# Attention and routing stage of a fused kernel: who issues the scatters, the counts, the state updates and the first transposes, and in which order

## The chip, the cores and the metric

The kernel runs on one core of a Trainium2 chip. The metric is the device time of one execution in microseconds (us). The engines are TensorE (PE), VectorE (DVE), ScalarE (ACT), GpSimd (POOL) and SyncE (SP), which here only issues DMAs.

## The reference, cut to what matters

Attention with a decay in place of a softmax (4 batches, 8 heads, 576 positions, 64 wide), then a layer of 8 experts of which each token takes the two with the best noisy logits, then a dense layer with h * cos(h).

```
ret = scores * Dmat[None, :, :, :]          # gamma ** (i - j), i >= j
x = (ret @ v).transpose(0, 2, 1, 3).reshape(B * S, H * D)      # 2304 x 512
noisy_logits = x @ w_gate + np.log1p(np.exp(x @ w_noise)) * noise
top2 = np.argpartition(-noisy_logits, 2, axis=1)[:, :2]
...
        h = np.maximum(x[mask] @ w1[e], 0.0)
        out[mask] += top2_w[mask, k, None] * (h @ w2[e])
...
h = x @ w_in
return ((h * np.cos(h)) @ w_out)
```

## The kernel before, in words

The first stage walks over 18 tiles `t` of 128 tokens (two sequences share nine tiles; within one, a running `state` carries what earlier tiles left). It is written as a software pipeline by step `s`. In step `s` PE computes the scores of tile `s` (line 1194), then for tile `s - 1` the part from the state (1209), the part from the tile itself (1217, counted in the semaphore `out_done`) and the state's growth (1225, `u_done`), then for tile `s - 2` the gate logits (1240) and the transposed rows (1245). DVE masks the scores (`scale`, line 909, result `ret`), and turns the growth into the new state (`carry`, 917). POOL multiplies q and k by decays (`q_dec`, 549, and `k_dec`, 557). ACT copies the output of a tile out of PSUM (`xT`, 634, and `x_sb`, 641). Scores of tile `t` need `ret` of tile `t - 1` done, since they write the same banks.

Routing runs beside it, in five groups of tiles (0-3, 4-7, 8-11, 12-14, 15-17). For a group, ACT does a softplus; DVE the first choice (8 small operations, lines 842-857), the second choice (7, lines 842-864) and the running sums (`sum_picks`, 869, one per tile, ending in `picked_done`); PE a small matmul that ranks the tokens (`count`, 1174-1179, ending in `counted`); and DVE the slots (`place_rows`, 881-895, ending in `pos_done`). Every one of these small DVE operations waits for the one before it. Tables such as `COUNT_AT` say in which step each runs. Then POOL scatters the rows of `x_sb` to the slots of their experts in memory, two indirect DMAs per tile (535), tiles 0 to 7 between its multiplications (`SCATTER_AT`), tiles 8 to 17 behind them. Eight transfers of zeros to the end of the experts' slots (`zero_tail`, 382) must have landed before the first scatter. SP issues the loads of qk, kv and raw weights in one fixed order; `load_qk(11)` waits until `q_dec` of tile 10 is done. Weights are split into a high and a low part as they come (ACT 608, DVE 820).

Behind the stage stands unit 0 of the experts. It is worked in two parts, its first two blocks of 128 slots (from tiles 0 to 7) ahead of the other three, which need all scatters done. Per block PE transposes the gathered rows (1270), ACT and DVE split them (`x_high` 650, `x_low` 999), then come the first product (`first1`, 1322) and the second (`first2`, 1334) for eight chunks of weights. `keep_clock(8)` (1261) is eight matmuls whose result nobody reads. After that the other units and the dense layer follow, 862 us that the change doesn't touch.

## Time and profile before

| | us |
|---|---|
| median of 3 runs | 1009.87 (1009.67 to 1010.83) |
| the profiled execution's own time | 1012.63 |
| its span, first to last instruction | 1010.7 |
| PE busy | 982.1 (97%) |
| DVE / ACT / POOL busy | 482.3 / 426.0 / 118.2 |

The profiled execution is 2.76 us longer than the median of the timed ones, and 1.93 us of it lie outside the span. Times in the trace count from the span's start. PE's weight loads run beside its matmuls and aren't added to its busy time. "Idle before" stands in brackets at a row's end, with what ended it.

### The profile page before, as it was taken

The numbers are of one execution on the slowest core, as the hardware profiler recorded it, in microseconds if no ns is written. First come the engines' busy times: TensorE is split into PE (matmuls) and PEld (weight loads), VectorE is DVE, ScalarE is ACT, GpSimd is POOL, SyncE is SP. The second block draws the span as 40 slices with busy tenths as digits, with TensorE's granted clock in tenths as the row PEclk, the third lists the DMA queues.
The fourth block names the chain that finished last, engine by engine and source line by source line (L and its number), as shares of the span: only waits on it lengthen the run. The fifth ranks groups of instructions, "written<-read, shape, count | busy, mean of one in ns | idle before, by whom it ended". The sixth has DMA issues, their size and how long they took to land.

```text
span 1010.7 us, 17316 instructions
## 1 busy us (share of the span) xinstructions
PE 982.1 (97%) x6116; PEld 887.9 (88%) x6116; DVE 482.3 (48%) x928; ACT 426.0 (42%) x779; POOL 118.2 (12%) x122
## 2 busy tenths in 40 slices
PE   8989799999999999999999989999999999999997
PEld 7878689899898989989899989999999999999996
DVE  3685464434333333333333466555555555555554
ACT  1442434333333333333334465455555555555554
POOL 4375520000000000000000131101000001010000
PEclk9996899999999999999999999999999999999999
DMA  9985552525445172544524452101010011011000
GB/s 364 308 304 208 194 202 84 197 96 177 156 129 203 62 257 75 185 147 145 187 74 148 159 192 95 42 32 42 21 52 21 21 52 37 36 34 29 31 0 32
DMA packets 64359, 122.02 MB, mean 121 GB/s; under 512 B 5696, under 2 KB 31552, under 8 KB 64320
## 3 DMA queue, kind: packets, MB, share of 16 engines
q1 hardware_dynamic: 58080, 101.05, 29.4%
q0 software_dynamic: 6240, 20.45, 6.1%
q8 instruction: 25, 0.41, 0.2%
q14 instruction: 14, 0.11, 0.0%
HBM read 83.73 MB, written 37.75 MB: 120 GB/s over the span
## 4 chain that ended last, share of the span: by engine, by line
PE 86%; DVE 4%; DMA 4%; issue 2%; SPq 1%; ACT 1%; another core or an unknown queue 1%; ACTq 0%; DVEq 0%
PE ps L1448 20%; PE ps L1467 20%; PE ps L1284 15%; PE ps L1302 14%; PE ps L1322 3%; PE ps L1334 3%; PE ps L1397 2%; PE ps L1409 2%; PE ps L1270 2%; DMA gath<-x_slots 2%; PE ps L1209 1%; PE ps L1240 1%; PE ps L1217 1%; DMA y_slots<-y_sb 1%; PE ps L1194 1%
## 5 line engine op out<-in xcount | busy, mean ns | idle before, releaser
L1284 PE MATMUL ps<-xs,w_hi 128*128 (+1 forms) x784 | 182.9, 312 | 0.0
L1020 DVE TENSOR_TENSOR w_lo<-raw,w_hi 128x1024 fp32r<-128x1024 f32 x48 | 58.8, 1225 | 170.0 <-ACT w_hi L665 170.0
L1284 PEld LDWEIGHTS ps<-xs,w_hi 128*128 128x128 f32 x784 | 133.1, 188 | 0.8
L1448 PE MATMUL ps<-x_hi,w_hi 128*128 (+1 forms) x384 | 130.8, 341 | 0.1
L1448 PE MATMUL ps<-x_hi,w_lo 128*128 (+1 forms) x384 | 129.1, 336 | 0.0
L1448 PE MATMUL ps<-x_lo,w_hi 128*128 (+1 forms) x384 | 129.1, 336 | 0.0
L790 ACT ACTIVATE turns<-ps 128x384 f32<-128x384 f32 x96 | 47.2, 491 | 183.7 <-PE ps L1448 183.6
L1284 PE MATMUL ps<-xs,w_lo 128*128 (+1 forms) x392 | 121.2, 309 | 0.0
L1144 DVE TENSOR_SCALAR turns<-turns 128x384 f32<-128x384 f32 x96 | 37.3, 388 | 167.6 <-ACT turns L790 167.6
L1467 PE MATMUL ps<-w_hi,g_hi 128*128 128x512 f32 x288 | 112.6, 391 | 2.1 <-DVE g_lo L1155 2.1
L1467 PE MATMUL ps<-w_hi,g_lo 128*128 128x512 f32 x288 | 113.3, 393 | 0.0
L1467 PE MATMUL ps<-w_lo,g_hi 128*128 128x512 f32 x288 | 113.3, 393 | 0.0
L665 ACT ACTIVATE w_hi<-raw 128x1024 fp32r<-128x1024 f32 x48 | 50.8, 1059 | 139.1 <-PE ps L1302 108.0
L1302 PE MATMUL ps<-w_hi,hs_lo 128*128 128x512 f32 x245 | 96.2, 393 | 0.0
L1302 PE MATMUL ps<-w_lo,hs_hi 128*128 128x512 f32 x245 | 96.2, 393 | 0.0
L1302 PE MATMUL ps<-w_hi,hs_hi 128*128 128x512 f32 x245 | 95.6, 390 | 0.0
L659 ACT ACTIVATE hs_hi<-ps 128x320 fp32r<-128x320 f32 x98 | 42.7, 437 | 80.9 <-PE ps L1284 80.9
L1448 PEld LDWEIGHTS ps<-x_hi,w_hi 128*128 128x128 f32 x384 | 72.1, 188 | 3.6 <-issue 0.5
L1448 PEld LDWEIGHTS ps<-x_hi,w_lo 128*128 128x128 f32 x384 | 72.1, 188 | 3.1
L1284 PEld LDWEIGHTS ps<-xs,w_lo 128*128 128x128 f32 x392 | 73.7, 188 | 0.8
L580 POOL DMA_INDIRECT y<-y_slots,pos_now x42 | 42.0, 1000 | 275.3 <-PE ps L1384 265.9
L1448 PEld LDWEIGHTS ps<-x_lo,w_hi 128*128 128x128 f32 x384 | 72.0, 188 | 0.0
(169 smaller groups left out, 1674.9 us busy)
## 6 DMA issues: line engine op xcount, KB each, us to landing
raw<-weights SPq DMA_DIRECT2D x80, 512.0 KB
y_slots<-zeros_sb SPq DMA_DIRECT2D x42, 256.0 KB, 3.7
gath<-x_slots SPq DMA_DIRECT2D x40, 256.0 KB, 3.5
y_slots<-y_sb SPq DMA_DIRECT2D x40, 256.0 KB, 2.1
qk<-qk SPq DMA_DIRECT2D x18, 512.0 KB
kv<-kv SPq DMA_DIRECT2D x18, 512.0 KB, 6.2
out<-out_sb SPq DMA_DIRECT2D x18, 256.0 KB, 2.1
x_slots<-zeros_sb SPq DMA_DIRECT2D x8, 256.0 KB, 8.2
```

The costliest lines, as they stand in the source:

```text
L580: nc.gpsimd.indirect_dma_start(out=y[j][:, :], out_offset=None, in_=y_slots, in_offset=bass.IndirectOffsetOnAxis(ap=pos_now[:, k, j:j + 1] ...
L659: nc.scalar.activation(hs_hi[:, par, half * HALF:(half + 1) * HALF], ps[5 + half][:, 0:HALF], ACT.Relu).then_inc(relu_done, 1)
L665: nc.scalar.activation(w_hi[:, f * CHUNK:(f + 1) * CHUNK], raw[:, f % 2, :], ACT.Copy).then_inc(hi_done, 1)
L790: nc.scalar.activation(turns[f % 2][:, :], h_bank(f)[:, 0:TB], ACT.Copy, scale=PER_TURN, bias=ROUND).then_inc(turn_done, 1)
L1020: tt(w_lo[:, at], raw[:, f % 2, :], w_hi[:, at].bitcast(F32), ALU.subtract).then_inc(split_done, 1)
L1144: ts(whole[:, :], whole[:, :], -ROUND, None, ALU.add).then_inc(whole_done, 1)
L1284: last_one = nc.tensor.matmul(ps[5 + half][:, 0:HALF], w[:, at:at + P], xs[:, bass.ds(g % 2, 1), a, k, half * HALF:(half + 1) * HALF].rear ...
L1302: last_one = nc.tensor.matmul(ps[j][:, :], a[:, f % 2, j * BLK:(j + 1) * BLK], w[:, at:at + DM], start=f == 0 and i == 0, stop=f == FE - 1 ...
L1322: last_one = nc.tensor.matmul(ps[5 + i % 2][:, 0:cols.stop - cols.start], w[:, at:at + P], xs[:, 0, a, k, cols], start=k == 0 and n == 0, ...
L1334: last_one = nc.tensor.matmul(ps[j][:, :], a[:, f % 2, j * BLK:(j + 1) * BLK], w[:, at:at + DM], start=f == 0 and n == 0, stop=f == FE - 1 ...
L1448: last_one = nc.tensor.matmul(h_bank(f)[:, 0:TB], w[:, cols], a[:, bass.ds(par, 1), k, :].rearrange("p a s -> p (a s)"), start=k == 0 and ...
L1467: last_one = nc.tensor.matmul(ps[j][:, :], a[f2 % 2][:, rows], w[:, cols], start=f2 == 0 and i == 0, stop=f2 == FT - 1 and i == 2)
```

## The change

Nothing is computed differently; the order changes on four engines, and two choices of PSUM bank.

- POOL: the two scatters of a tile no longer follow each other behind both multiplications; one stands behind `q_dec` and one behind `k_dec`, and all of them run one step earlier (from step 9). The zeros go out up to two steps earlier.
- DVE: `carry` comes right behind `scale`; the second choice, the sums and the slots follow it. `place_rows` of groups 0, 1, 2 stands one step earlier (8, 12, 16), that of group 3 behind `x_low` of unit 0; the first choice of group 4 moves behind `x_low` too.
- PE: `count` of groups 0, 1, 2 moves from the end of steps 8, 12, 16 to right behind their scores. The transposes of x for unit 0's first two blocks move from behind the stage into its last step, ahead of the logits of tile 17. `keep_clock` does four matmuls in place of eight. `count` of group 4 moves one product later.
- ACT: `x_high` of these blocks moves ahead of the last softplus.

The tables and the banks:

```
-COUNT_AT = {8: 0, 12: 1, 16: 2, 18: 3}
-PLACE_AT = {9: 0, 13: 1, 17: 2, 19: 3}
-SCATTER_AT = {10: (0,), 11: (1,), 12: (2,), 13: (3,), 14: (4,), 15: (5,), 16: (6,), 17: (7,)}
-ZERO_AT = {t: t - 3 for t in range(3, 3 + E)}
-SPLIT_AT = {4: 0, 5: 1, 8: 2, 9: 3, 12: 4, 16: 5}
+COUNT_AT = {8: 0, 12: 1, 16: 2}
+PLACE_AT = {8: 0, 12: 1, 16: 2}
+SCATTER_AT = {9: 0, 10: 1, 11: 2, 12: 3, 13: 4, 14: 5, 15: 6, 16: 7}
+ZERO_AT = {3: (0,), 4: (1,), 5: (2, 3), 6: (4, 5), 7: (6,), 8: (7,)}
+SPLIT_AT = {4: 0, 5: 1, 8: 2, 9: 3, 13: 4, 16: 5}
...
-            return ps[j] if isinstance(g, int) and g == 0 else ps[7]
+            return ps[j if j < FRONT[0] else j + 3] if isinstance(g, int) and g == 0 else ps[7]
...
+        def h_first(f, part_no):
+
+            return ps[(2, 5)[part_no] + f % 2]
```

POOL's walk over the tiles:

```
+                if t == 9:
+                    pool.wait_ge(x_zero, 16 * E)
+                if t in SCATTER_AT:
+                    scatter_rows(SCATTER_AT[t], 0)
                 if c < CB - 1:
...
-                if t == 10:
-                    pool.wait_ge(x_zero, 16 * E)
-                for n in SCATTER_AT.get(t, ()):
-                    scatter_rows(n)
+                if t in SCATTER_AT:
+                    scatter_rows(SCATTER_AT[t], 1)
```

ACT's step:

```
                 if t == NT - 1:
+                    for j in range(FRONT[0]):
+                        x_high(0, j)
                     softplus(NG - 1)
```

DVE's walk, and what follows it:

```
-            for s in range(NT + 2):
+            for s in range(NT + 1):
                 if s < NT:
                     scale(s)
-                if s in SECOND_AT:
-                    second_choice(SECOND_AT[s])
-                if s in PLACE_AT:
-                    place_rows(PLACE_AT[s])
                 if 0 < s <= NT and (s - 1) % CB < CB - 1:
                     carry(s - 1)
                 if s in SECOND_AT:
+                    second_choice(SECOND_AT[s])
                     sum_picks(SECOND_AT[s])
+                if s in PLACE_AT:
+                    place_rows(PLACE_AT[s])
...
-            first_choice(NG - 1)
             for j in range(FRONT[0]):
                 x_low(0, j)
+            place_rows(NG - 2)
             h_low_first(0, 0)
+            first_choice(NG - 1)
+            h_low_first(1, 0)
             second_choice(NG - 1)
             sum_picks(NG - 1)
-            h_low_first(1, 0)
+            h_low_first(2, 0)
             place_rows(NG - 1)
```

PE's step, and what follows the stage:

```
+                if s in COUNT_AT:
+                    count(COUNT_AT[s])
                 t, c = s - 1, (s - 1) % CB
...
                 t = s - 2
+                if t == NT - 1:
+                    for j in range(FRONT[0]):
+                        transpose_x(0, j)
...
-                if s in COUNT_AT:
-                    count(COUNT_AT[s])
+                if t == NT - 2:
+                    count(NG - 2)
...
-                if i == 1:
-                    pe.wait_ge(ranked, NG - 1)
...
-            for j in range(FRONT[0]):
-                transpose_x(0, j)
-            keep_clock(8)
+            keep_clock(4)
             first1(0, 0)
             first1(1, 0)
             first2(0, 0)
             first1(2, 0)
-            count(NG - 1)
             first2(1, 0)
+            count(NG - 1)
```

The order on PE around step 12, first before (from the last matmuls of step 11; the lines are those named above):

```order
L1217 MATMUL ps<-ret,kv 64x128 x8
L1225 MATMUL ps<-kv,k_dec 64x64 x8
L1240 MATMUL ps<-wg,xT 128x16 x4
L1245 MATMUL ps<-table_sb,xT 128x128 x4
L1174 MATMUL ps<-picked,table_sb 128x32
L1176 MATMUL ps<-before_sum,table_sb 128x32
L1179 MATMUL ps<-before_sum,table_sb 128x8
L1194 MATMUL ps<-qk 128x128 x8
L1209 MATMUL ps<-q_dec,state 64x128 x8
L1217 MATMUL ps<-ret,kv 64x128 x8
```

And after the change, whose lines are numbered some twenty higher (1212 the scores, 1183 to 1188 the count, 1229 and 1237 the tile's output, 1245 the state's growth, 1263 and 1268 logits and rows):

```order
L1212 MATMUL ps<-qk 128x128 x8
L1183 MATMUL ps<-picked,table_sb 128x32
L1185 MATMUL ps<-before_sum,table_sb 128x32
L1188 MATMUL ps<-before_sum,table_sb 128x8
L1229 MATMUL ps<-q_dec,state 64x128 x8
L1237 MATMUL ps<-ret,kv 64x128 x8
L1245 MATMUL ps<-kv,k_dec 64x64 x8
L1263 MATMUL ps<-wg,xT 128x16 x4
L1268 MATMUL ps<-table_sb,xT 128x128 x4
L1212 MATMUL ps<-qk 128x128 x8
```

The three matmuls of the count have gone from behind the rows of step 12 to between its scores and the output of tile 11.

POOL's list in the middle of the scatters, first before, one tile's four instructions and what follows:

```order
L535 DMA x_slots<-x_sb,pos_x 20480x512 [waits x_done,pos_done]
L535 DMA x_slots<-x_sb,pos_x 20480x512
L549 TENSOR_TENSOR q_dec<-qk,attn_table 128x512 [waits out_done,qk_in0]
L557 TENSOR_TENSOR k_dec<-kv,attn_table 128x512 [waits u_done,kv_in0]
L535 DMA x_slots<-x_sb,pos_x 20480x512 [waits x_done,pos_done]
L535 DMA x_slots<-x_sb,pos_x 20480x512
L549 TENSOR_TENSOR q_dec<-qk,attn_table 128x512 [waits out_done,qk_in1]
```

And after (552 is `q_dec`, 564 `k_dec`, 538 the scatter):

```order
L552 TENSOR_TENSOR q_dec<-qk,attn_table 128x512 [waits out_done,qk_in2]
L538 DMA x_slots<-x_sb,pos_x 20480x512 [waits x_done,pos_done]
L564 TENSOR_TENSOR k_dec<-kv,attn_table 128x512 [waits u_done,kv_in2]
L538 DMA x_slots<-x_sb,pos_x 20480x512 [waits x_done,pos_done]
L552 TENSOR_TENSOR q_dec<-qk,attn_table 128x512 [waits out_done,qk_in0]
L538 DMA x_slots<-x_sb,pos_x 20480x512 [waits x_done,pos_done]
L564 TENSOR_TENSOR k_dec<-kv,attn_table 128x512 [waits u_done,kv_in0]
```

The two multiplications no longer stand side by side; a scatter stands ahead of each.

The end of the stage on PE, first before, from step 18 on:

```order
L1209 MATMUL ps<-q_dec,state 64x128 x8
L1217 MATMUL ps<-ret,kv 64x128 x8
L1240 MATMUL ps<-wg,xT 128x16 x4
L1245 MATMUL ps<-table_sb,xT 128x128 x4
L1174 MATMUL ps<-picked,table_sb 128x24
L1176 MATMUL ps<-before_sum,table_sb 128x24
L1240 MATMUL ps<-wg,xT 128x16 x4
L1245 MATMUL ps<-table_sb,xT 128x128 x4
L1270 MATMUL ps<-table_sb,gath 128x128 x8
L1261 MATMUL ps<-w_hi 128x512 x8
L1322 MATMUL ps<-xs,w_hi 128x256
```

And after (1197 is the transposes of x, 1284 the four matmuls of `keep_clock`, 1334 the first product):

```order
L1229 MATMUL ps<-q_dec,state 64x128 x8
L1237 MATMUL ps<-ret,kv 64x128 x8
L1263 MATMUL ps<-wg,xT 128x16 x4
L1268 MATMUL ps<-table_sb,xT 128x128 x4
L1183 MATMUL ps<-picked,table_sb 128x24
L1185 MATMUL ps<-before_sum,table_sb 128x24
L1197 MATMUL ps<-table_sb,gath 128x128 x8
L1263 MATMUL ps<-wg,xT 128x16 x4
L1268 MATMUL ps<-table_sb,xT 128x128 x4
L1284 MATMUL ps<-w_hi 128x512 x4
L1334 MATMUL ps<-xs,w_hi 128x256
```

The transposes of x now stand ahead of the logits and rows of tile 17, which come between them and the first product.

## Rows read from the trace of the kernel before

**Rows 1.** Windows view of six stretches; per engine busy us (instructions).
```profile
core 0: us, PE busy (x) PEld busy (x) DVE busy (x) ACT busy (x) POOL busy (x), PEclk, DMA share, GB/s
36.94:42.02 5.08, 5.08 (x78) 4.55 (x77) 4.67 (x15) 1.63 (x4) 1.85 (x2) 1.00 1.03 356
61.41:106.42 45.01, 38.67 (x467) 34.80 (x467) 28.88 (x68) 15.86 (x27) 29.23 (x28) 0.81 0.68 241
76.79:92.97 16.18, 14.76 (x122) 13.16 (x124) 9.46 (x30) 2.35 (x4) 7.67 (x8) 0.50 0.59 210
106.42:122.89 16.47, 10.30 (x76) 8.76 (x76) 7.01 (x34) 5.15 (x10) 10.36 (x11) 0.79 0.56 213
122.89:148.74 25.85, 24.43 (x163) 22.11 (x163) 17.02 (x66) 8.16 (x15) 9.53 (x9) 1.00 0.51 187
148.74:1010.70 861.96, 850.71 (x4592) 770.00 (x4592) 394.24 (x675) 373.45 (x691) 44.32 (x49) 1.00 0.29 96
```

**Rows 2.** Timeline of PE, 36.9 to 58 us: start, length, engine, line, operation.
```profile
36.94 1.16 PE L1194 MATMUL ps<-qk 64*128 64x128 f32 x16
...
39.97 0.64 PE L1225 MATMUL ps<-kv,k_dec 128*64 128x64 f32 x16
...
47.15 0.39 PE L1176 MATMUL ps<-before_sum,table_sb 128*128 128x32 f32 x2
...
56.33 1.16 PE L1194 MATMUL ps<-qk 64*128 64x128 f32 x16
```

**Rows 3.** Waits of PE, 0 to 125 us: total us, times, longest.
```profile
PE ps L1194 <- DVE ret L909: 4.5, 2, 3.0
...
PE ps L1209 <- DVE state L917: 3.1, 3, 1.6
```

**Rows 4.** Timeline of DVE, 59 to 93 us.
```profile
60.52 2.77 DVE L846 TENSOR_TENSOR hots<-t_b,code 128x32 f32<-128x32 f32 x1
...
63.90 0.76 DVE L869 TENSOR_TENSOR before_sum<-before_sum,picked 128x8 f32<-128x8 f32 x4
...
69.79 4.03 DVE L820 TENSOR_TENSOR w_lo<-raw,w_hi 128x1024 fp32r<-128x1024 f32 x1 [2.62 <-ACT w_hi L608]
...
91.08 0.18 DVE L862 SCALAR_TENSOR_TENSOR t_c<-hots,logit 128x32 f32<-128x32 f32 x1
...
92.42 0.19 DVE L864 TENSOR_TENSOR picked<-hots 128x32 f32<-128x32 f32 x1
```

**Rows 5.** Timeline of POOL, 50 to 64 us.
```profile
50.83 1.27 POOL L549 TENSOR_TENSOR q_dec<-qk,attn_table 128x512 f32<-128x512 f32 x1 [2.81 <-PE ps L1217]
...
59.96 0.97 POOL L535 DMA_INDIRECT x_slots<-x_sb,pos_x  x1 [0.30 <-issue]
60.95 1.29 POOL L549 TENSOR_TENSOR q_dec<-qk,attn_table 128x512 f32<-128x512 f32 x1
62.17 1.06 POOL L557 TENSOR_TENSOR k_dec<-kv,attn_table 128x512 f32<-128x512 f32 x1
63.40 1.01 POOL L535 DMA_INDIRECT x_slots<-x_sb,pos_x  x1 [0.17 <-issue]
```

**Rows 6.** Timeline of the SP queue, 50 to 146 us.
```profile
52.17 0.33 SPq L389 DMA_DIRECT2D qk<-qk  x1
...
141.31 2.23 SPq L423 DMA_DIRECT2D gath<-x_slots  x5
```

**Rows 7.** Timeline of PE, 112 to 149 us.
```profile
119.32 2.51 PE L1261 MATMUL ps<-w_hi 128*128 128x512 f32 x8
...
144.48 1.03 PE L1270 MATMUL ps<-table_sb,gath 128*128 128x128 f32 x8
145.27 0.47 PE L1334 MATMUL ps<-w_hi,hs_hi 128*128 128x512 f32 x1
```

**Rows 8.** Timeline of ACT, 106 to 123 us.
```profile
111.92 0.60 ACT L634 ACTIVATE xT<-ps 128x512 f32<-128x512 f32 x1 [5.02 <-remote]
```

**Rows 9.** Timeline of DVE, 109 to 123 us.
```profile
117.62 0.20 DVE L886 TENSOR_TENSOR pos_hot<-hots,ps 128x48 f32<-128x48 f32 x1 [7.64 <-remote]
```

More of the change, by code:

```diff
@@ L417, in _ @@
                     load_chunk(SPLIT_AT[t + 1], SPLIT_AT[t + 1])
-                if t in ZERO_AT:
-                    zero_tail(ZERO_AT[t])
+                for e in ZERO_AT.get(t, ()):
+                    zero_tail(e)
             load_chunk(FE - 2, FE - 2)
@@ L529, in _, with scatter_rows @@
             nc.gpsimd.memset(zeros_sb[:, :], 0.0).then_inc(rows_zero, 1)
-            def scatter_rows(t):
+            def scatter_rows(t, k):
                 pool.wait_ge(pos_done, group_of(t) + 1)
                 pool.wait_ge(x_done, t + 1)
-                for k in range(2):
-                    nc.gpsimd.indirect_dma_start(
-                        out=x_slots, out_offset=bass.IndirectOffsetOnAxis(ap=pos_x[:, k, t:t + 1], axis=0),
-                        in_=x_sb[t][:, :], in_offset=None).then_inc(rows_early if t < EARLY else rows_late, 16)
+                nc.gpsimd.indirect_dma_start(
+                    out=x_slots, out_offset=bass.IndirectOffsetOnAxis(ap=pos_x[:, k, t:t + 1], axis=0),
+                    in_=x_sb[t][:, :], in_offset=None).then_inc(rows_early if t < EARLY else rows_late, 16)
             for t in range(NT):
@@ L624, in softplus, with x_high @@
                     nc.scalar.activation(sin_ready[:, :], tab("half_pi"), ACT.Exp)
+            def x_high(g, j):
+                act.wait_ge(tx_done, TPU * g + j + 1)
+                nc.scalar.activation(
+                    xs[:, bass.ds(g % 2, 1), 0, :, j * BLK:(j + 1) * BLK].rearrange("p a k s -> p (a k) s"),
+                    x_bank(g, j)[:, :].rearrange("p (k s) -> p k s", k=KD_TILES), ACT.Copy).then_inc(xs_hi_done, 1)
             def step(s):
@@ L679, in relu_first @@
                     act.wait_ge(p2_done, i - 1)
-                nc.scalar.activation(hs_hi[:, f % 2, cols], ps[5 + i % 2][:, 0:cols.stop - cols.start], ACT.Relu
+                nc.scalar.activation(hs_hi[:, f % 2, cols], h_first(f, part_no)[:, 0:cols.stop - cols.start], ACT.Relu
                                      ).then_inc(relu_done, 1)
@@ L1049, in _ @@
             for f in range(2, FE):
[L1050 removed]
+                if f > 2:
+                    h_low_first(f, 0)
                 if f == 2:
@@ L1181, in count, with transpose_x @@
                 last_one.then_inc(counted, 1)
+            def transpose_x(g, j):
+                pe.wait_ge(gath_in[j], 16 * g + 16)
+                if not isinstance(g, int) or g > 0:
+                    pe.wait_ge(xs_done, TPU * g + j)
+                for k in range(KD_TILES):
+                    last_one = nc.tensor.transpose(x_bank(g, j)[:, k * BLK:(k + 1) * BLK], gath[j][:, k * P:(k + 1) * P],
+                                                   ident)
+                last_one.then_inc(tx_done, 1)
             def step(s):
@@ L1263, in _ @@
             pe.wait_ge(split_done, 1)
-            def transpose_x(g, j):
-                pe.wait_ge(gath_in[j], 16 * g + 16)
-                if not isinstance(g, int) or g > 0:
-                    pe.wait_ge(xs_done, TPU * g + j)
-                for k in range(KD_TILES):
-                    last_one = nc.tensor.transpose(x_bank(g, j)[:, k * BLK:(k + 1) * BLK], gath[j][:, k * P:(k + 1) * P],
-                                                   ident)
-                last_one.then_inc(tx_done, 1)
             def product1(g, f):
@@ L1339, in first2 @@
                         last_one.then_inc(y_ready, 1)
-            for j in range(FRONT[0]):
-                transpose_x(0, j)
-            keep_clock(8)
+            keep_clock(4)
             first1(0, 0)
@@ L1347, in _ @@
             first1(2, 0)
+            first2(1, 0)
             count(NG - 1)
-            first2(1, 0)
             for f in range(3, FE):
```

14 lines of the change are left out of this document (4 added, 10 removed).

## The prediction

> **What bounds the kernel now.** I read the windows view first: the stage that the change touches, and its hand-over to the experts. Behind 148.74 us there are 862 us with PE busy for 850.7 and a granted clock of 1.00 [rows 1]; nothing that the change moves stands there, so its time counts only if PE reaches that point earlier. In the stage PE is the bound while nothing disturbs it: one step lasts 5.08 us, with PE busy for 5.08 [rows 1]. From 61.41 to 106.42, steps 12 to 17, it took 45.01 us. Six undisturbed steps and two counts would take 6 x 5.08 + 0.5 + 0.7 = 31.7; a count costs about 0.5 or 0.7 (one starts its second matmul pair at 47.15 and takes 0.39 more, beside the first pair; the one of step 12 has three) [rows 1, 2]. So 13.3 us were lost, in two forms. The waits view has PE waiting for `ret` (4.5 us in 2 waits) and for `state` (3.1 in 3) [rows 3]. And behind the longest of these, 3.0 us up to 76.79, the granted clock is 0.50 from 76.79 to 92.97, the lower level of 1.2 GHz, while PE is busy for 14.76 of 16.18 us [rows 1]: at 2.4 GHz that work is 7.4 us, so the slow stretch alone cost 7.4.
>
> What made DVE late is seen in its timeline beside POOL's. A small operation (`hots`) that starts at 60.52 takes 2.77 us, where its like takes 0.19; a split that starts at 69.79 takes 4.03 [rows 4]. POOL runs a scatter to 60.93, `q_dec` to 62.24 and `k_dec` to 63.23 without a gap; 63.29 is where DVE's operation ends, and only then comes POOL's next scatter, after 0.17 us [rows 5]. DVE is shut out while POOL's multiplications follow each other, and already in the scatter ahead of them. The sums at 63.90 (0.76 for four) run beside a scatter unhindered [rows 4, 5]: a scatter that no multiplication follows doesn't shut it out.
>
> The rule for this is in the Trainium skill, SBUF — State Buffer, Who interferes with whom: an operation of VectorE with two SBUF inputs and one of GpSimd exclude each other, and the one that starts first has the ports for its whole instruction. By that rule alone the longest hold is one multiplication, 1.29 us, and each of the two later counts below would wait 0.5 us less (1.1 us held instead of 1.6); the gain would be 8.4 us in place of my 7.4. This trace differs, with 2.77 us and 4.03 us, so the sum goes by the trace.
>
> **The change part by part.**
>
> *GpSimd alternates.* The hold of 2.77 us falls apart into two: scatter and `k_dec`, scatter and `q_dec`. Each lasts from the middle of the scatter (0.4 us into it: the operation at 60.52 was 0.56 in) to the end of the multiplication, 0.57 + 1.06 = 1.6 and 0.57 + 1.29 = 1.9 us [rows 4, 5]. No single hold is as long as before, but together they are 3.5 us of a cycle of some 4.7 (60.95 + 1.22 + 1.23 + two scatters of 1.27), where it was 2.9. DVE's free stretches are 0.6 us each, enough for two or three small operations.
>
> *State first.* The waits for `state`, 3.1 us, go: the small operations now stand behind `carry`. `ret` stands as before, except that the slots of group 1 now end ahead of the long `ret` of tile 13. With the shorter holds I give the six steps their 31.7 us, that is 13.3 us back, and charge the waits that come anew.
>
> *Counts behind the scores.* This is the cost. The count needs the sums, and these now come after `carry`. In a step the state's growth starts 3.03 us in (39.97 - 36.94) [rows 2]; `carry` ends 4.1 us in. `q_dec` begins where the tile's output ends, some 3.4 us in, and lasts 1.27 [rows 5], so the second choice gets going 4.6 us in. It takes 1.53 (91.08 to 92.61) and the sums 0.76 [rows 4]: 6.9, or 1.9 into the next step, while PE is through with the scores at 1.1 (the length in [rows 2]). So the count of group 0, where no scatters run, makes PE wait 0.9. For groups 1 and 2 a scatter and `k_dec` come in between: DVE gets 0.6 us in, is held for 1.6 and ends 3.5 us into the step: 2.4 us of waiting, for each. Lower bound 0.9; upper bound 5, if POOL runs late and a second and third hold are met. I take 2.4 twice. Together 5.7. PE has nothing else to do meanwhile, since it works in order; behind the count are queued the output of the tile, and with it `xT` on ACT and POOL's next `q_dec`.
>
> *Scatters a step earlier.* POOL at tile 9 now waits for the slots of group 0 (about 49.3: step 8 starts at 42.02, the wait of 0.9 and the count of 0.5 put the growth of tile 7 at 47.1, then come `carry` and seven operations like those of the choices). Behind that wait stand one scatter, `k_dec`, another scatter and `q_dec` of tile 10, 1.27 + 1.05 + 1.27 + 1.3 = 4.9 us. That `q_dec` ran from 50.83 and released SP's `load_qk(11)` at 52.17; the scores of tile 11 started at 56.33, 4.2 us later [rows 2, 5, 6]. Now it goes out at 54.3, and the scores start at 58.4 instead of 56.33 + 0.9 (the wait already charged): 1.2 us more. Bounds 0 and 3.5.
>
> *Zeros earlier, split later.* At most two transfers of 256 KB more stand ahead of the loads of tiles 7 to 10. PE didn't wait for any of these, and I charge nothing; if the cover is gone it is 1 us. For `ret` and scores that a hold or the split delays I add 0.9.
>
> *The end of the stage.* From 106.42 to the first product at 122.89 it took 16.47 us, with PE busy for 10.30 at a clock of 0.79 [rows 1]. In the new order PE does there step 18 without scores (1.1) and growth (0.5), 3.5 us, with a count, 0.5; eight transposes, 0.8 (144.48 to 145.27); the logits and rows of tile 17, 1.5 (what a step has behind its growth); and four matmuls of `keep_clock`, 1.2 (eight took 2.51) [rows 2, 7]. That is 7.5 us, and the split of x on ACT and DVE hides behind the last two. So up to 9.0 us are to be had. But part of the 16.47 was no order of ours: ACT sat idle for 5.02 us before `xT` of tile 17, and DVE 7.64 before the slots of group 3, both put down to "remote", that is to nothing that the trace shows as running [rows 8, 9]; the matmuls that they waited for stand in the timeline some us before. POOL was issuing eight scatters in a row then, and will again. Bounds for this lateness 0 and 7.6; I keep the middle of the two rows, 6.3. That leaves 2.7 us.
>
> *Behind it.* The slots of group 4 come one `first2` later (1.4 us), and with them the last scatters and the five loads that SP issued at 141.31; PE took them up at 144.48 without waiting [rows 6, 7]. Between 0 and 1.4, I take 0.8.
>
> **The sum.** 13.3 - 5.7 - 1.2 - 0.9 + 2.7 - 0.8 = 7.4 us. The profiled execution took 1012.63, so 1005.2; it is 2.8 above the median of the timed runs, which gives 1002.4.
>
> **The rivals.**
>
> *The slow clock comes again.* A wait of 3.0 us led to it before, one of 1.6 at 62.5 did not. My waits at the counts are 2.4, in between, and there are two. For it: the wait for `ret` up to 76.79 wasn't alone, others preceded it; against: steps on either side are fully busy. Price 7.4, the whole gain: 1009.8.
>
> *The picks are cut to pieces (slower).* The place is the second choice of groups 1 and 2. If POOL runs a little late, the free stretches of 0.6 us let two or three of its eleven operations through at a time, and each count waits 5 us. Two times 2.6 more, and such a wait surely brings the slow clock: 7.4 - 5.2 - 7.4 = -5.2, or 1015.1. It decides as soon as the clock falls and the two counts together wait 2 us longer than the 4.8 that I say. Against it: POOL depends on PE's output, so while PE waits, POOL runs dry and frees DVE.
>
> *The lateness at the end is gone.* The transposes need only the loads, and logits stand behind them. Then 6.3 more: 996.1. Against it: the same scatters in a row.
>
> **How the numbers follow.** Forecast 0.40 (its own range 999 to 1006), slow clock 0.32, cut picks 0.14, lateness gone 0.09, and 0.05 for the rest. The range from 997 to 1012 leaves out about 0.18. A change within 0.2%, 2 us, can't be told from none by this measurement. The forecast and the third case are faster, and of the slow-clock case, which lies at the edge of that band, a third is faster, half the same and the rest slower: faster 0.62, same 0.17, slower 0.21.
>
> **What would show it.** Right: no operation of DVE above 2 us between 50 and 95; PE's waits at 1183 some 1 and twice 2.4 us; no wait at 1229 for `state`; a clock of 1.00 to 95; the first product at about 115. Wrong: a wait above 3 us at a count with a clock of 0.5 behind it; a start of the first product later than 120; or new waits behind 149, where I expect the same 862 us.

## The result, and the profile after

The kernel after took 1015.11 us (median of 6 runs, 1013.07 to 1016.94) against 1009.79 for the kernel before (6 runs): a ratio of 1.0047, 95% interval 1.0033 to 1.0062. In a second set of runs it was 1.0046 (1.0028 to 1.0065). The forecast was 1002.4, in a range up to 1012; the time lies outside it, on the slower side. The profiled execution of after took 1014.13 us, with a span of 1012.2.

The windows view of after, first the stages of [rows 1] (steps 8 to 11, steps 12 to 17, the end of the stage, the first part of unit 0, the rest), then three stretches at a low clock. The columns are the length, the busy time of PE, PE's weight loads, DVE, ACT and POOL, then the granted clock, the DMA share and GB/s:

```profile
41.76:65.79 24.03, 21.09 (x277) 18.61 (x276) 13.64 (x40) 9.85 (x16) 14.53 (x13) 0.93 0.69 251
65.79:108.05 42.26, 36.03 (x467) 32.13 (x466) 28.81 (x72) 14.98 (x26) 25.92 (x23) 0.88 0.68 239
108.05:120.56 12.51, 9.70 (x73) 8.35 (x73) 5.06 (x24) 5.43 (x12) 5.23 (x6) 0.76 0.45 176
120.56:148.90 28.34, 25.40 (x164) 22.32 (x162) 18.36 (x74) 8.41 (x16) 12.11 (x12) 0.98 0.52 183
148.90:1012.20 863.30, 851.09 (x4592) 769.85 (x4592) 394.60 (x675) 373.46 (x691) 45.57 (x49) 1.00 0.30 96
59.15:63.70 4.55, 4.55 (x48) 4.00 (x50) 1.29 (x2) 0.00 (x0) 4.13 (x4) 0.62 1.02 383
69.70:73.40 3.70, 3.70 (x36) 3.35 (x37) 0.64 (x2) 0.00 (x0) 0.00 (x0) 0.57 0.42 169
93.25:100.90 7.65, 5.97 (x53) 5.29 (x55) 3.79 (x14) 0.00 (x0) 1.74 (x2) 0.56 0.65 236
```

Steps 8 to 11 took 24.03 us, where from 42.02 to 61.41 it was 19.39 [rows 1]. Steps 12 to 17 took 42.26 instead of 45.01, the end of the stage 12.51 instead of 16.47, the first part of unit 0 28.34 instead of 25.85, the rest 863.30 instead of 861.96 [rows 1]. Ahead of step 8, which begins at 41.76 instead of 42.02, 0.26 us were won, so this is 4.64 - 2.75 - 3.96 + 2.49 + 1.34 - 0.26 = 1.5 us, the difference of the two spans. The one long stretch at half clock is gone, and three short ones have come: 0.62, 0.57 and 0.56 are mixtures of the levels 1.2 and 2.4 GHz.

PE's waits from 41 to 110 us (total, times, longest), the line before the colon, and two of them in its timeline:

```profile
PE ps L1183 <- DVE before_sum L875: 4.6, 3, 2.2
PE ps L1212 <- DVE ret L915: 2.3, 2, 2.0
PE ps L1212 <- DMA qk<-qk: 2.3, 1, 2.3
```

```profile
69.20 0.41 PE L1183 MATMUL ps<-picked,table_sb 128*128 128x32 f32 x2 [2.24 <-DVE before_sum L875]
...
93.25 1.31 PE L1212 MATMUL ps<-qk 64*128 64x128 f32 x16 [1.96 <-DVE ret L915]
```

The waits for `state` [rows 3] are gone. In their place stand three at the counts (L1183: 0.65, 2.24 and 1.67 us) and one for the load of `qk` of tile 11. DVE's longest operations between 50 and 95:

```profile
65.89 1.78 DVE L850 TENSOR_TENSOR t_b<-t_a,table_sb 128x32 f32<-128x32 f32 x1
...
82.32 2.48 DVE L826 TENSOR_TENSOR w_lo<-raw,w_hi 128x1024 fp32r<-128x1024 f32 x1 [2.21 <-ACT w_hi L614]
...
89.79 2.00 DVE L852 TENSOR_TENSOR hots<-t_b,code 128x32 f32<-128x32 f32 x1
```

The 2.77 and 4.03 us of [rows 4] are gone too, but a choice of 0.19 us still takes 1.8 or 2.0, and there are more of these.

The hand-over, in POOL's timeline (eight scatters, then six for group 3 and six for group 4; the first of each six is shown), SP's and PE's:

```profile
120.13 0.95 POOL L538 DMA_INDIRECT x_slots<-x_sb,pos_x  x1 [5.83 <-DVE pos_x L901]
...
131.34 1.77 POOL L538 DMA_INDIRECT x_slots<-x_sb,pos_x  x1 [3.93 <-DVE pos_x L901]
```

```profile
141.46 2.23 SPq L427 DMA_DIRECT2D gath<-x_slots  x5
```

```profile
144.28 1.25 PE L1197 MATMUL ps<-table_sb,gath 128*128 128x128 f32 x8 [1.53 <-DMA gath<-x_slots]
...
148.90 0.45 PE L1334 MATMUL ps<-xs,w_hi 128*128 128x384 f32 x1 [1.41 <-DVE xs L1005]
```

POOL waits 5.83 us for the slots of group 3 and 3.93 for those of group 4. The gather loads go out at 141.46, where it was 141.31 [rows 6], and PE now waits 1.53 us for them. So the 2.3 us by which the first product begins earlier are lost at the second part, which starts at 148.90 instead of 148.74. Of the 2.49 us by which the first part is longer, 1.53 are this wait, and 0.97 are a longer busy time of PE (25.40 against 24.43), at a clock of 0.98 in place of 1.00.

### The profile page after: what moved, and what is told of

Its sections match the earlier page's. It is cut to its first block, busy times and chain, and to the rows that moved or that the text cites. A ratio compares the mean times of both kernels' runs of the same rounds, so it can differ in the third digit from the quotient of the medians.

```text
span 1012.2 us, 17321 instructions
## 1 busy us (share of the span) xinstructions
PE 982.5 (97%) x6112; PEld 886.8 (88%) x6112; DVE 480.5 (47%) x928; ACT 425.7 (42%) x779; POOL 122.1 (12%) x122
## 4 chain that ended last, share of the span: by engine, by line
PE 83%; DMA 5%; issue 4%; DVE 3%; POOL 2%; SPq 1%; ACT 1%; ACTq 0%; POOLq 0%; DVEq 0%
PE ps L1458 20%; PE ps L1477 19%; PE ps L1298 15%; PE ps L1316 14%; DMA gath<-x_slots 2%; PE ps L1197 2%; PE ps L1334 2%; PE ps L1407 2%; PE ps L1346 2%; POOL x_slots L538 2%; PE ps L1419 2%; DMA y_slots<-y_sb 1%; PE ps L1237 1%; PE ps L1229 1%; PE ps L1212 1%
```

## The experiments

The runs were made in five sets, each on one chip and beside runs of the kernel before on that chip, so each ratio stands for itself. The medians of before in them were 1010.39 us (b_pool, b_tail, a_table, a_pool), 1003.46 (before2, t_chain, b_chain, a_q11), 1011.18 (after2, a_cend, a_chain, t_alt), 1010.70 (a_warm, b_cnt, t_altz, best1) and 1010.01 (a_warm2, best2). A difference of 0.001 in a ratio is 1 us. Where two ratios come from different sets, the chip differs as well as the kernel, and the text says what the traces show beside them.

**A second trace of before.** The forecast was built on one trace whose own time lay 2.8 us above the median.

> The kernel before, once more, for a second trace. If the first trace was a usual execution, the span is 1010 to 1011 and steps 12 to 17 take 45 us with 16 us at half clock; if it was a long one (its own time is 2.8 us above the median), the span is 1007 to 1009 and these steps take 41 to 43.

It took 1005.18 us, with a span of 1003.3, on a chip where the median of before was 1003.46. The span lies below both of the expected ones. Its windows: steps 12 to 17, the end of the stage, the first part of unit 0, the rest, and the only stretch at half clock:

```profile
61.80:103.03 41.23, 33.87 (x467) 30.53 (x467) 28.83 (x68) 15.87 (x27) 29.32 (x28) 0.92 0.75 267
103.03:113.39 10.36, 8.30 (x77) 7.04 (x77) 7.26 (x34) 5.15 (x10) 7.92 (x9) 1.00 0.70 256
113.39:139.11 25.72, 24.31 (x162) 21.95 (x163) 16.96 (x66) 8.16 (x15) 11.98 (x12) 1.00 0.58 210
139.11:1003.30 864.19, 851.07 (x4592) 769.88 (x4592) 394.43 (x675) 373.28 (x691) 44.59 (x49) 1.00 0.29 96
77.22:86.77 9.55, 7.19 (x77) 6.46 (x77) 5.51 (x18) 1.74 (x3) 5.44 (x6) 0.64 0.56 203
```

Steps 12 to 17 took 41.23 us, within the second of the expected ranges. This alone doesn't settle the question, since the chip is another one and this execution too was longer than the median there. But b_tail and b_chain below leave the order of these steps as in before, and b_tail ran on a chip of the usual speed, in an execution as long as its median (1010.93 and 1011.0 us). Its steps 12 to 17:

```profile
61.73:103.16 41.43, 34.09 (x467) 30.71 (x467) 29.03 (x68) 15.86 (x27) 29.15 (x28) 0.92 0.72 261
```

In b_chain they took 40.96. The undisturbed length was 31.7, so a usual execution loses 9.3 to 9.7 us there and not 13.3. In before2 the slow stretch is 9.55 us long and not 16.18, and costs 7.19 x (1 - 0.64) = 2.6 us and not 7.4. The rest varies by itself: 864.19 here, 861.96 before, 863.30 in after.

**One part alone, and one part undone.** b_pool and b_tail put a part into before; a_table and a_pool take one out of after.

```diff
 b_pool: before, tile loop of GpSimd
+                if t in SCATTER_AT:
+                    scatter_rows(SCATTER_AT[t], 0)
                 if c < CB - 1:
...
+                    scatter_rows(SCATTER_AT[t], 1)
 a_pool: after, the same lines taken out, and both scatters behind k_dec
 a_table: after with
+COUNT_AT = {8: 0, 12: 1, 16: 2, 18: 3}   (at the steps' ends)
+PLACE_AT = {9: 0, 13: 1, 17: 2}
+SCATTER_AT = {10: 0, 11: 1, ... 17: 7}   (zeros and splits in the steps of before too)
 b_tail: before with the diff's parts behind step 17 on PE, ACT and DVE
```

> Before, with one part of the change alone: at tiles 10 to 17 each scatter stands behind one multiplication, the tables of before kept. Timetable theory (the loss of 5.3 us comes from counts, slots and scatters a step earlier): this stays near before, 1007 to 1011, DVE's operations of 2.77 and 4.03 us gone, the half clock not longer than the 16 us of before. Alternation theory (the rival: scatters between the multiplications cost GpSimd or DVE more than they free): 1013 to 1016, with DVE's picks cut into more pieces and PE waiting for ret more than 4.5 us.

> Before, with the end of the stage alone changed: the x tiles of unit 0 transposed ahead of the last logits, their banks, four instead of eight clock-keeping products, rows placed and experts chosen behind the first slots of unit 0. Timetable theory: 1008 to 1011; the first product begins 1 to 5 us earlier than 122.89, and the second part of unit 0 still begins near 148.9, since the rows of group 4 reach their slots no earlier. Hand-over theory (rival: the new end is the loss): 1013 to 1016, the second part at 151 or later.

> After, with the tables of before (counts at the end of steps 8, 12, 16, places and scatters a step later); alternation, state first and the new end stay. Timetable theory: 1006 to 1010, 5 to 9 us less than after; no wait for the load of qk at step 11, no wait of PE at a count, half clock under 10 us between 41 and 107. Alternation or hand-over theory: stays at 1013 to 1016.

> After, with both scatters of a tile behind both multiplications again, one step earlier than before. Timetable theory: 1013 to 1017, the waits at the counts and for the load of qk at step 11 stay, unless the second multiplication, now ahead of the wait for the slots, lets the load go out by 53 (then 2 us less). Alternation theory: 1009 to 1011.

Measured: b_pool 1.0027 (1.0013 to 1.0042), b_tail 1.0010 (0.9998 to 1.0022), a_table 1.0042 (1.0026 to 1.0057), a_pool 1.0038 (1.0019 to 1.0058). My theory at that point, that the earlier tables are the loss, fell in its simple form: without them (a_table) the kernel stays slow, and alternation alone costs 2.8 us. The new end costs nothing that can be measured, and gains nothing. State first had no run of its own; what is left for it, 1.0042 less the 1.0027 and 1.0010 of the other two parts, is 0.0005, within the error. But a_pool shows that alternation isn't the whole loss either: after without it is at best 0.9 us faster, which is within the error. Against what was expected, PE does wait at a count in a_table, 2.5 us. In b_tail the first product began at 117.76, 5.1 us earlier than in the first trace of before, and the second part at 147.17.

**The counts.**

```diff
 a_cend: after
-                if s in COUNT_AT:          (behind the scores)
-                    count(COUNT_AT[s])
                 if t == NT - 2:
                     count(NG - 2)
+                if s in COUNT_AT:          (at the end of the step)
+                    count(COUNT_AT[s])
 b_cnt: before, with the opposite move
```

> After, with its counts again at the end of steps 8, 12 and 16 and nothing else undone: places in the same step and scatters a step early stay. Timetable theory, if the counts' waits are its price: no wait of PE at a count, steps 8 to 16 in 55 to 58 us, 3 to 6 us less than after, ratio to before 0.998 to 1.002. If the early scatters are its price (slots of group 0 ahead of the multiplications of tile 9): 1.003 to 1.006 still.

> Before, with the counts of steps 8, 12 and 16 behind the scores and nothing else changed. Counts theory (they alone are 5.8 us between after and a_cend): PE waits 0.5 to 4 us at each of three counts, ratio 1.002 to 1.006. If the counts cost only beside the early scatters: 0.999 to 1.001.

> The kernel after, once more, for a second trace and a second ratio. Timetable theory (PE waits for the picks at the counts of steps 8, 12 and 16, each time with half clock behind it; in the three traces with these tables steps 8 to 16 take 61.2 to 61.9 us, without them 54.6 to 58.8): ratio 1.003 to 1.006 on any chip, steps 8 to 16 in 60 to 63 us. If the loss belonged to the chip's late releases at the end of the stage, the ratio would be 0.998 to 1.002 where releases are on time.

The second trace of after is like the first: steps 8 to 16 took 61.15 us, and PE's waits at the three counts 4.6. a_cend gave 0.9991 (0.9975 to 1.0008) beside 1.0046 for after on the same chip: the place of three counts is 5.8 us (1010.89 against 1016.72). Its windows, steps 8 to 11 and 12 to 17, then steps 8 to 17 of after2 in one:

```profile
42.20:65.29 23.09, 20.80 (x278) 18.71 (x277) 15.74 (x38) 9.86 (x16) 14.10 (x12) 0.93 0.69 252
65.29:102.36 37.07, 33.46 (x467) 30.04 (x467) 30.61 (x72) 15.67 (x26) 27.14 (x25) 0.95 0.83 298
```

```profile
42.26:108.49 66.23, 57.41 (x744) 51.32 (x743) 41.62 (x111) 24.83 (x42) 40.57 (x35) 0.90 0.68 245
```

Steps 12 to 17 take 37.07 instead of 42.26. Over steps 8 to 17 a_cend takes 60.16 us and after2, on the same chip, 66.23. PE's work is the same but for its place, and its busy time is 54.26 against 57.41, its idle time 5.90 against 8.82. So of the 6.1 us between the two traces about half, 3.15, is half clock and the other half, 2.92, is waiting. Steps 8 to 16 took 52.86 us in a_cend, less than was expected, though it isn't free of the count's wait: PE waits 1.47 us at the one of step 16.

a_table has its counts at the steps' ends too, and it took 1.0042. It differs from a_cend in that slots, scatters, zeros and one split stand in the steps of before. So with the counts at the ends the early scatters seem to gain 5 us, not to cost any; the two ratios are from two chips, but their intervals are well apart. The traces don't show where: steps 8 to 17 take 60.39 us in a_table and 60.16 in a_cend. This stays open.

In the kernel before, the same move (b_cnt) costs little: 1.0012 (0.9996 to 1.0028), which fits neither end of what was expected; its one long wait at a count is 2.10 us, at step 12:

```profile
65.12 0.41 PE L1174 MATMUL ps<-picked,table_sb 128*128 128x32 f32 x2 [2.10 <-issue]
```

The window behind it, from 65.12 to the scores of step 13:

```profile
65.12:69.87 4.75, 4.75 (x66) 4.32 (x66) 1.57 (x3) 0.60 (x1) 4.24 (x4) 1.00 0.81 318
```

The clock stays at 1.00, where behind the wait of 2.24 us in after it was 0.57. So a count is dear where the clock falls behind it. That it falls in after because other waits stand near (for `qk` at step 11, for `ret` at step 16) is a guess which no run tests alone.

**Wait or clock.** The same counts, with products that nobody reads ahead of them, as long as the waits.

```diff
 a_warm: after
+FILL = {8: 5, 12: 18, 16: 16}    (a_warm2: {8: 1, 12: 5, 16: 4})
                 if s in COUNT_AT:
+                    for i in range(FILL[s]):
+                        nc.tensor.matmul(logit_bank(COUNT_AT[s])[:, 256:512], ident, attn_table[:, 0:256], ...)
                     count(COUNT_AT[s])
```

> After, with 5, 18 and 16 products of 128x256 on TensorE ahead of the counts of steps 8, 12 and 16, into columns that nobody reads, which fill 0.5, 2.0 and 1.7 us of the waits there. If half clock behind the waits is the price: no half clock at steps 12 and 16, 3 to 5 us less than after, ratio 1.000 to 1.002. If the waits themselves are: no change, 1.004 to 1.006.

> After, filled again ahead of its counts, now with 1, 5 and 4 products. In a_warm the filling was too long: its 39 products took 0.43 us each (two passes of 0.21), 16.8 us in all where the waits are 4.6 to 5.7. Now 0.4, 2.1 and 1.7 us. If half clock behind the waits is the price: none at steps 12 and 16, ratio 1.000 to 1.002. If the waits themselves are: 1.004 to 1.006.

a_warm gave 1.0149 and says nothing about the question: I had taken a product for 0.11 us, and it is 0.43 at full clock. a_warm2 gave 1.0027 (1.0016 to 1.0037), between the two expectations; the interval overlaps those of after (from 1.0028 and 1.0033 up), and the chip is another one. Its waits and two windows, behind the counts of step 12 and of step 16:

```profile
PE ps L1213 <- DVE ret L916: 2.4, 2, 2.0
PE ps L1213 <- DMA qk<-qk: 2.0, 1, 2.0
PE ps L1184 <- DVE before_sum L876: 0.2, 1, 0.2
```

```profile
69.70:75.00 5.30, 5.28 (x74) 4.85 (x76) 2.85 (x10) 1.02 (x2) 1.26 (x1) 1.00 0.47 175
91.60:100.00 8.40, 7.75 (x52) 6.63 (x54) 4.44 (x15) 0.00 (x0) 2.36 (x3) 0.59 0.56 185
```

At step 12 the wait is down to 0.2 us and the clock stays at 1.00. At step 16 it falls all the same, behind the wait of 2.0 us for `ret` at 92.25. At step 12 the filling takes about as long as the wait did, so what is gained there is clock: from the scores of step 12 to those of step 16 it takes 26.28 us, in after 27.46, 1.2 us less, where half clock in the window behind 69.70 had cost after 3.70 x 0.43 = 1.6. At step 16 the four products themselves run at the low clock, from 94.25 to 97.82, and take 3.6 us where the wait was 1.67; so half of the gain is lost again. Over steps 8 to 17 the trace is only 0.8 us shorter than after's (65.47 against 66.29), and whether the ratio's 1.9 us is this gain isn't shown.

**The load of qk of tile 11.** It waits for `q_dec` of tile 10, though the last reader of its buffer is that of tile 8.

```diff
 a_q11: after
-sp.wait_ge(q_dec_done, updates(t - 3) + (1 if (t - 3) % CB == CB - 1 else 0))
+sp.wait_ge(q_dec_done, updates(t - 3))
```

> After, with the load of qk of tile 11 waiting for the q_dec of tile 8, the last reader of its buffer, and not for that of tile 10. Timetable theory: the wait of 2.3 us at the scores of step 11 and the half clock behind it go, 1011 to 1013.5. Alternation or end theory: the time is taken up by the next wait, 1014 to 1016.

1.0042 (1.0029 to 1.0055), on the chip where before took 1003.46: no gain that shows beside the 1.0046 of after on another chip. The wait of 2.3 us is gone, and steps 8 to 11 take 22.11 us instead of 24.03; but at step 12 PE now waits 1.74 us for `ret` and 3.24 at the count, and steps 12 to 17 take 44.89 instead of 42.26. The next wait took its place, as the rival said.

**The hand-over.** The choices, the count and the places of group 4 ahead of DVE's and PE's work on the first slots.

```diff
 t_chain: b_tail, DVE                     PE
             place_rows(NG - 2)                       first2(0, 0)
+            first_choice(NG - 1)         +           count(NG - 1)
             h_low_first(0, 0)                        first1(2, 0)
-            first_choice(NG - 1)                     first2(1, 0)
-            h_low_first(1, 0)            -           count(NG - 1)
             second_choice(NG - 1)
             sum_picks(NG - 1)
+            h_low_first(1, 0)
-            h_low_first(2, 0)
             place_rows(NG - 1)
 b_chain: before, and a_chain: after, with the same aim
```

> The run with the new end alone (b_tail), and in it the choices of group 4 ahead of the first slots' h_low, its count before the third product, its places before the third h_low. Join theory (what ends the first part of unit 0 is the chain last rows, picks, places, six scatters, gather; in all six traces it takes 28.1 to 29.7 us from the last rows to the second part): the places end near 125 instead of 129.6, the second part begins 3 to 4 us earlier, median 1006.5 to 1008.5. Rival (the join is PE's own work, and the loss of the new end lies in the clock behind its four clock-keeping products): 1010 to 1012, no change.

> Before, with the choices of group 4 ahead of h_low of the first slots, its count before first2 of chunk 0 and its places before h_low of chunk 1. Join theory: in the kernel before PE's work and the gather chain end together (no wait of PE for the gather, 144.48), so an earlier gather alone gives 0 to 1.5 us: 1008.5 to 1010.5. If the chain alone set the join: 1006 to 1008.

> After, with the choices, count and places of group 4 in the order of t_chain. If the join is set by the gather chain in after as well: 2 to 3 us less than after, ratio 1.001 to 1.003; if by PE's own work or by GpSimd's queue of scatters behind the slots of group 3: no change, 1.004 to 1.006.

t_chain gave 0.9986 (0.9973 to 0.9998), just faster than before, and 0.0024 below b_tail, whose interval from another chip touches its own; b_chain 1.0007 (0.9996 to 1.0018); a_chain 1.0043 (1.0029 to 1.0057), no change against after. Windows of b_tail and then of t_chain, each the end of the stage and the first part of unit 0:

```profile
103.16:117.76 14.60, 8.82 (x73) 7.52 (x73) 5.04 (x24) 4.29 (x9) 7.48 (x8) 0.82 0.52 202
117.76:147.17 29.41, 26.46 (x164) 22.89 (x162) 18.98 (x77) 8.90 (x17) 12.53 (x12) 0.97 0.47 177
```

```profile
102.27:109.48 7.21, 7.17 (x72) 6.42 (x73) 4.76 (x22) 3.91 (x8) 5.57 (x6) 1.00 0.76 287
109.48:137.52 28.04, 25.19 (x164) 21.78 (x162) 19.63 (x79) 9.61 (x18) 14.56 (x14) 1.00 0.58 211
```

The first part takes 29.41 and 28.04 us where [rows 1] has 25.85: with the new end PE is early and waits for the gather (0.89 us in b_tail, 0.62 in t_chain). In before PE's work and the gather end together, so an earlier gather alone (b_chain) brings nothing. In after the twelve scatters of groups 3 and 4 wait for places that come after `x_low`, and reordering group 4 alone (a_chain) doesn't help. The windows of 14.60 and 7.21 us can't be compared, since they are from two chips (below); nor is the 0.0024 between t_chain and b_tail shown to be the new order's alone. Beside before2 on its own chip t_chain takes 35.25 us from step 18 to the second part and before2 36.08.

**Why alternation costs.** t_alt adds it to t_chain; t_altz also writes the zeros as early as after does.

> The faster version t_chain (ratio 0.9986), with alternation of multiplications and scatters at tiles 10 to 17 added. Alternation theory (b_pool: 1.0027 alone; k_dec of tile 10 behind a scatter, PE waits 1.1 us for it and state 1.5 us longer): 1.0005 to 1.002. If b_pool's loss was its longer half clock by chance of that chip: 0.998 to 0.9995, as t_chain.

> t_alt with the zeros of the slots written as early as in after. Gate theory (alternation with the tables of before costs 3.9 us because k_dec of tile 10 stands behind the first scatter, and that behind the zeros, which land 6.3 us after q_dec): first scatter near 54, k_dec of tile 10 by 56, no wait of PE for k_dec, ratio 0.998 to 1.000. If the pieces into which alternation cuts VectorE's picks cost it (1.31, 2.01, 1.77, 2.48 us instead of one of 2.73): 1.001 to 1.003 still.

t_alt: 1.0025 (1.0011 to 1.0039), 0.0039 above t_chain and above the range expected; steps 8 to 17 take 63.33 us, in t_chain 60.37, and all of the difference is a longer busy time of PE (56.72 against 53.29), that is half clock. Its POOL and PE:

```profile
51.01 1.27 POOL L552 TENSOR_TENSOR q_dec<-qk,attn_table 128x512 f32<-128x512 f32 x1 [2.55 <-PE ps L1234]
58.60 1.16 POOL L538 DMA_INDIRECT x_slots<-x_sb,pos_x  x1 [6.32 <-ACT x_sb L655]
59.80 1.05 POOL L564 TENSOR_TENSOR k_dec<-kv,attn_table 128x512 f32<-128x512 f32 x1
```

```profile
60.90 0.69 PE L1242 MATMUL ps<-kv,k_dec 128*64 128x64 f32 x16 [1.18 <-POOL k_dec L564]
```

`k_dec` of tile 10 stands behind the first scatter, and PE waits 1.18 us for it. This looked like the cause, and t_altz took it away: its first scatter starts at 54.32 and PE no longer waits for `k_dec`. It still gave 1.0034 (1.0017 to 1.0050). That theory fell; the other one had named 1.001 to 1.003. DVE's timeline in t_altz at steps 11 and 12:

```profile
58.08 2.02 DVE L849 TENSOR_TENSOR t_a<-logit,top 128x32 f32<-128x32 f32 x1
...
60.57 1.77 DVE L852 TENSOR_TENSOR hots<-t_b,code 128x32 f32<-128x32 f32 x1
...
65.31 1.77 DVE L850 TENSOR_TENSOR t_b<-t_a,table_sb 128x32 f32<-128x32 f32 x1
...
67.79 0.42 DVE L923 TENSOR_TENSOR state<-ps,attn_table 128x256 f32<-128x256 f32 x1
```

Each multiplication that stands alone holds a choice for 1.8 to 2.0 us, and `state`, which in this order comes behind the second choice, ends at 68.21; PE starts on it at 68.36, after 3.38 us. In t_chain PE waits 1.52 us for `state` at that place. Steps 8 to 17 take 62.86 us in t_altz, 2.5 more than in t_chain, and here all of it is waiting (PE busy for 53.35).

**The parts that gained, together.** best1 is a_cend with the load of a_q11 and the order of t_chain; best2 is best1 without alternation.

> A version put together from the parts that gained: after with its counts at the steps' ends (a_cend, 0.9991), the load of qk of tile 11 behind q_dec of tile 8, and the choices, count and places of group 4 as in t_chain. If the wait of 2.3 us and the half clock at step 11 go and the join follows: 0.995 to 0.998. If the next wait takes their place: 0.998 to 1.000.

> best1 (0.9981) without alternation: both scatters of a tile behind both multiplications, one step early. Pieces theory (each multiplication that stands alone holds a choice of VectorE for 1.8 to 2.0 us, a pair holds one for 2.6 to 2.8): fewer long picks at steps 11, 12, 15, ratio 0.994 to 0.997. If alternation costs nothing a step early (a_pool 1.0038 against after 1.0047): 0.997 to 0.9995.

best1: 0.9981 (0.9963 to 0.9999), where the next wait was to take the place of the first. best2: 0.9914 (0.9901 to 0.9928), 1001.97 us against 1010.01: 8.0 us faster than before, more than either theory had said, and, by the ratios of two sets, 6.7 us faster than best1. DVE's timeline in best1 and then best2, choices of group 1:

```profile
59.07 2.00 DVE L849 TENSOR_TENSOR t_a<-logit,top 128x32 f32<-128x32 f32 x1
...
61.56 1.78 DVE L852 TENSOR_TENSOR hots<-t_b,code 128x32 f32<-128x32 f32 x1
...
66.31 1.78 DVE L850 TENSOR_TENSOR t_b<-t_a,table_sb 128x32 f32<-128x32 f32 x1
...
68.57 2.00 DVE L870 TENSOR_TENSOR picked<-hots 128x32 f32<-128x32 f32 x1
70.60 0.77 DVE L875 TENSOR_TENSOR before_sum<-before_sum,picked 128x8 f32<-128x8 f32 x4
```

```profile
58.11 2.83 DVE L860 TENSOR_TENSOR t_b<-t_c,noise_sb 128x32 f32<-128x32 f32 x1
...
63.86 1.82 DVE L866 SCALAR_TENSOR_TENSOR t_c<-hots,logit 128x32 f32<-128x32 f32 x1
...
67.07 0.84 DVE L873 TENSOR_TENSOR before_sum<-before_sum,picked 128x8 f32<-128x8 f32 x4
```

The choices begin at 58.0 in both. With alternation four of them are held for 1.8 us and more, 7.56 together, and the sums end at 71.37. Without it two are held, for 4.65, and the sums end at 67.91. Steps 12 to 17 of best1 and then of best2:

```profile
64.81:102.30 37.49, 34.99 (x467) 31.29 (x467) 31.29 (x76) 15.39 (x26) 26.38 (x23) 0.91 0.75 252
63.76:95.87 32.11, 31.60 (x466) 28.60 (x467) 28.27 (x76) 15.27 (x26) 25.74 (x23) 1.00 0.84 297
```

In best2 the clock is 1.00 and PE is idle for 0.5 us: the six steps take 32.11 us, close to the undisturbed 31.7. Over steps 8 to 17 best1 takes 59.63 us and best2 53.32, so the traces bear out the 6.7 us of the ratios. Of these 6.3 us, 4.95 are busy time of PE at the lower clock (55.89 against 50.94) and 1.36 are waiting. In after itself, with the counts behind the scores, taking alternation out gained nothing clear (a_pool). So alternation has no fixed price: the longer chain on DVE was paid as half clock in t_alt, as waiting in t_altz, as both in best1, and not visibly in after.

## Why the prediction was wrong

**The step that failed first: "with the shorter holds I give the six steps their 31.7 us, that is 13.3 us back".** Two things were wrong in it. The 13.3 us were those of one execution, 2.8 us longer than the median, with a slow stretch of 16.18 us; other traces with the same order have 9.3 to 9.7 us to give. Taking the 2.8 off at the end didn't repair that, since it let the whole gain of the long execution stand. With 9.5 in place of 13.3, and nothing taken off for a long execution, the same sum gives a gain of 3.6 us and 1006.2: this explains 3.8 of the 12.7 us between 1002.4 and 1015.11. The other 8.9 are in the steps that didn't become undisturbed, and in the stages around them. In after, PE waits 6.2 us in steps 12 to 17, where I charged 5.7 (4.8 at the counts, 0.9 for `ret` and scores), and half clock adds 36.03 - 31.7 = 4.3, where I charged none. It is this term, put at nothing, that failed: the price of the low clock, 4.3 us there and 1.7 in step 11. So nothing was left: 42.26 us against 41.23 in the second trace of before.

The reading of the waits was loose too. Of the 4.5 us for `ret` in [rows 3], 1.57 stand at 8.12, far ahead of these steps. In the steps themselves PE was idle for 45.01 - 38.67 = 6.3 us, and the other 7.0 of the 13.3 were half clock. More than half of what was to be won was clock, and the only term that could have cost it again was left to a rival.

**Alternation.** The sizes were right: holds of 1.6 and 1.9 us were predicted, 1.78 and 2.00 measured, and their sum per tile was put at 3.5 us against 2.9 for the pair. But I charged nothing for it and counted the shorter single hold as the gain. It is the sum that counts, since the choices are a chain on DVE and a count, a `ret` or a `state` waits for its end. (The cycle that I put at 4.7 us is 1.22 + 1.23 + 2 x 1.27 = 5.0 by its own terms, which makes the free stretches 0.75 us, not 0.6; it changes nothing in the sum.) Alternation alone costs 2.8 us in before (b_pool), 3.9 on t_chain, 6.7 between best1 and best2, the last two across two chips, and in after at most 0.9 (a_pool).

**Counts behind the scores.** The waits were forecast well: 0.9, 2.4 and 2.4, measured 0.65, 2.24 and 1.67 (5.7 and 4.6 in sum). What wasn't charged is the clock behind them, my rival of 0.32. In after it fell behind a wait of 2.29, one of 2.24 and one of 1.96 (with the count's 1.67 inside the slow stretch); not behind the 0.65. So two of the three falls follow waits for `qk` and `ret`, which I had put at 1.2 and 0.9 us. Keeping the counts at the steps' ends gives 5.8 us back (a_cend), about half of it clock. The rival "slow clock" had the mechanism and nearly the size: 7.4 us in one stretch, where it came to 6.0 in steps 8 to 17 in three; its total of 1009.8 was too low since the rest of the forecast was. The rival "picks cut to pieces" named 1015.1, the time that came, but that is luck in good part: its mechanism came only in part. The pieces are there, but the counts didn't wait 5 us each, and the rest of its sum was made up by half clock and the hand-over.

**Scatters a step earlier.** 1.2 us for the load of `qk` of tile 11; it was 2.29, and half clock in the next 4.55 us cost 4.55 x 0.38 = 1.7 more. Undoing it alone gains nothing (a_q11). Whether the early scatters as such cost or gain is open: beside counts at the steps' ends they seem to gain (a_cend and a_table).

**State first.** Right: no wait for `state` is left in after.

**The end of the stage.** 2.7 us were forecast, 3.96 came. The low clock stayed there too, 0.76 in this stage, and PE waited 1.59 us for `xT` of tile 17. My 7.5 us for PE's own work there were right: on the chip without the late releases t_chain took 7.21 and a_q11 6.92. The first product began at 120.56, past the 120 that I had named as a sign of being wrong.

**Behind it.** 0.8 us; it was 2.49. I had looked only at how much later the slots of group 4 come relative to the first product, not at the fact that PE's work and the gather ended together in before (no idle time ahead of the transposes at 144.48, [rows 7]). What brings the first product forward then makes PE wait, 1.53 us here, until the gather comes earlier too; the other 0.97 is PE's longer busy time.

**The length of a hold.** The Trainium skill (SBUF — State Buffer, Who interferes with whom) has the first of the two engines keep the ports for its whole instruction. The single holds of 1.78 and 2.00 us are longer than the multiplications of 1.05 and 1.27 behind them, as I took from [rows 4, 5]; the trace goes beyond the rule, and it was not the step that failed.

In sum: the profiled execution was forecast at 1005.2 and took 1014.13, 8.9 us more, by stages: 2.5 in steps 8 to 11, 4.9 in steps 12 to 17, 1.7 in the first part of unit 0, 1.3 in the rest, less 1.3 at the end of the stage and 0.3 ahead of step 8.

What stays open: why the clock fell behind some waits and not behind others as long; what the early scatters are worth by themselves; and why the last 862 us differ by up to 2.2 us between executions.

## What to carry to other kernels

Before a stall is turned into a gain, look whether it is there in a second execution; a profiled run that lies above the median has its excess somewhere, and here it lay in the very stretch that the change was to mend. Give the low clock a term of its own in the sum, for the gain and for the cost, and not only a rival. Where two engines shut each other out, count the sum of the holds on the chain that someone waits for, not the longest one: splitting a pair of GpSimd's multiplications made more holds and a later end. And a sync point on PE that moves forward is paid twice where the clock falls behind it: once as the wait, and once as half clock, here in about equal parts.

## What the runs showed of the hardware

- The same kernel took 1003.46 us on one chip and 1010.01 to 1011.18 on four others. The second trace of before is from the first of these: its end of the stage took 10.36 us at a clock of 1.00 (103.03:113.39 above), where [rows 1] have 16.47 at 0.79, with the idle times put down to "remote" in [rows 8, 9]. No version but before was timed on both kinds of chip. The nearest pair, a_q11 there with 1.0042 and after elsewhere with 1.0046 and 1.0047, agrees.
- A small operation of VectorE that meets a lone multiplication of GpSimd behind a scatter takes up to 1.8 or 2.0 us, and one that meets a pair up to 2.73 to 2.83.
- The granted clock fell behind waits of PE of 2.0 to 2.3 us, in after three times between 59 and 101. Behind the count of step 12 it stayed at 1.00 once the wait there was filled with products. But the length of one wait doesn't decide it: it stayed at 1.00 behind 2.10 us in b_cnt and behind 2.11 at 66.79 in b_pool, and it fell behind 1.06 us at 57.91 in best1 (0.75 from 57.91 to 64.81) and, some 2 us later, behind 1.18 at 60.90 in t_alt (0.67 from 60.90 to 66.26).
